# RWKV-style attention and two MLPs on one core: phase 1 without a loop, attention pieces moved

## Chip, cores, metric

One NeuronCore of a Trainium2 chip runs the whole program. The metric is the device time of one execution in microseconds (us), the median over several runs.

## What is computed

Four batches, eight heads, 768 steps, head size 48. The attention is a recurrence over steps, with a decay `w` per channel:

```python
for t in range(S):
    cur = einsum('bhd,bhe->bhde', u * k[t], v[t])
    y[t] = einsum('bhd,bhde->bhe', r[t], state + cur)
    state = w[t][..., None] * state + einsum('bhd,bhe->bhde', k[t], v[t])
x = y as (3072 tokens, 384)
h = x @ w_in                          # 384 x 2048
x = knee(h) @ w_out                   # 2048 x 384; knee: h above 1, 0 below -1, (h+1)^2/4 between
out = (silu(x @ w_gate) * (x @ w_val)) @ w_out2   # 384 x 1536, 1536 x 384
```

## The kernel before

The 3072 tokens are cut into 8 halves (NG = 8; two per batch) of 384 tokens (T), each half into 3 windows of 128. Every large product is taken three times, as hi x hi, hi x lo and lo x hi of operands split into two parts of type fp32r.

**Phase 1** does the first MLP of half g while the attention of half g+1 is woven in. It has 16 slots per half, one for each 128 rows of the hidden layer. In slot j TensorE does `tile_in` of tile j+2 (nine products of 384 columns, line 1042, into PSUM bank `hid[j % 2]`) and `tile_out` of tile j (nine more, line 1066, into `acc`). The tile in between goes through ScalarE (relu and square, lines 701 and 703), VectorE (`gate`, line 926), ScalarE (`ghi`, line 694) and VectorE (`glo`, line 919). In its slot j VectorE does `glo` of tile j+1, `gate` of tile j+2, and then whatever else the slot holds, in that order. `tile_out` waits for `glo` of its tile, and `tile_in` of tile j+4 for `gate` of tile j+2.

**The attention of a half** is a list of 18 pieces, FILLS: for each window KT (k transposed), AT (the products of k and r; two entries, done together), ST (state), Y (output) and XT (output transposed). They use three PSUM banks in turn. WIN_SLOTS puts two entries into each of slots 4 to 12: TensorE does the first between `tile_in` and `tile_out`, the second behind `tile_out`. The next half's `tile_in`, in slot 14, needs all three XT.

Ahead of the pieces stand, on VectorE, the scaling of k and r by the decays (`scale_k`, `scale_r`, lines 856 and 864: 4 instructions in slot 1 and 4 in slot 2) and `diag_sum` (line 868, slot 3). `diag_sum` reads what GpSimd made of r, k and u by two products (`diag_products`, lines 622 and 626); behind it GpSimd does `diag_values` (line 633). The scans of the decays for half g+2 (`scan_pair`, 4 instructions a pair of heads) are VectorE's in slots 9 to 12.

**Loads** are all issued by SyncE, in a fixed order: `load_w(g+2)` when half g+1 is scaled; `load_rest(g+2)` (k and r by channel, then r, k, v by token) when all 18 pieces of half g+1 are done and its y are out; then the store of half g's result. GpSimd's first product waits for r and k by token.

Halves 0 to 5 of phase 1 run in a loop of three rounds of two halves, on every engine (SyncE and GpSimd have loops of their own); halves 6 and 7 are written out. **Phase 2** (the second MLP) has 12 slots per half, with a loop of three rounds of two halves too; it does not change. The attention and the pieces of half 0, with the conversion of the first MLP's weights, come before phase 1.

Of the kernel before, what the change touches and what calls it, by code (L numbers as in the profile page):

```python
# [38 lines left out]
NG = B * S // T  # L39
# [17 lines left out]
NF = len(FILLS)  # L57
# [2 lines left out]
OPS_CHECK = 4  # L60


SCALE_SLOTS = {1: (0, 1), 2: (2, 3)}
DIAG_SLOT = 3
WIN_SLOTS = {4 + i: (2 * i, 2 * i + 1) for i in range(NF // 2)}

CHECK_SLOTS = {5: 0, 6: 1}
SUM_SLOT = 8
SCAN_SLOTS = {9: 0, 10: 1, 11: 2, 12: 3}

CHECK_FILLS = {0: 0, 1: 1}
SCAN_FILLS = {3: 0, 4: 1, 5: 2, 6: 3}
# [10 lines left out]
def build_program(nc, w_d, kd_d, rd_d, rn_d, kn_d, vn_d, u_d, cst_d, w1i_d, w1o_d, w2g_d, w2v_d,  # L83
                  w2o_d, rs_d, ks_d, vs_d, ws_d, us_d, out_d, x2_d, ys_d):
    ctx = ExitStack()
    with ctx:
# [170 lines left out]


        def phase1(e, slot):
            with e.Fori(0, NG // 2 - 1) as b:  # L260
                for hf in range(2):
                    for j in range(J1):
                        slot(b * 2 + hf, j, hf, True, True)
            for g in (NG - 2, NG - 1):
                for j in range(J1):
                    slot(g, j, g % 2, g == NG - 2, False)

        def phase2(e, slot):
            for j in range(J2):
# [208 lines left out]
        def _(e):  # L478
# [65 lines left out]
            def half(g, after_next):  # L544

                if after_next:
                    load_w(g + 2)
                    load_rest(g + 2)
                wait(M["ea", 1], g * 2 + 4)
                wait(M["ed", 1], g + 2)  # L550

                e.dma_start(half_of(x2_d, g), stage[:, :, :]).then_inc(M["st", 1], 16)

            with e.Fori(0, NG // 2 - 1) as b:
                for hf in range(2):
                    half(b * 2 + hf, True)

            wait(fill, NG * NF)
            wait(xl_out, NG * NW)
# [38 lines left out]
        @block.gpsimd  # L598
        def _(e):

            for i in range(2):
                e.memset(att[i][:, :, :], 0.0).then_inc(zero_p, 1)
            e.memset(st[:, :, :], 0.0).then_inc(zero_p, 1)
            e.memset(seed[:, :], 0.0).then_inc(zero_p, 1)

            def split_lo(c, buf, raws, lo, whi_s, wlo_s):
                n = len(raws)
                e.wait_ge(whi_s, c + 1)
                e.wait_ge(raws[c % n], 16 * (c // n + 1))
                e.tensor_tensor(lo[0], buf[:, c % n, :], lo[1].bitcast(F32), ALU.subtract).then_inc(wlo_s, 1)  # L610

            def w1_lo(c):
                if (c + 1) % DVE_LO == 0:
                    return
                t = w1i if c % 2 == 0 else w1o
                split_lo(c, ring, raw, (t[1][:, c // 2, :], t[0][:, c // 2, :]), whi, wlo)

            def diag_products(g):

                e.wait_ge(ld["rn"], (g + 1) * 16)  # L620
                e.wait_ge(ld["kn"], (g + 1) * 16)
                e.tensor_tensor(rk[:, :, :], rk[:, :, :], kn[:, :, :], ALU.mult).then_inc(diag_p, 1)
                e.wait_ge(diag_p, g * 3 + 1)
                e.wait_ge(ld["u"], 16)
                u_b = uu[:, :].rearrange("p (a n) -> p a n", a=1).to_broadcast([P, NW, DM])
                e.tensor_tensor(rk[:, :, :], rk[:, :, :], u_b, ALU.mult).then_inc(diag_p, 1)

            def diag_values(g):

                e.wait_ge(diag_d, g + 1)  # L630
                e.wait_ge(ld["vn"], (g + 1) * 16)
                d_b = dg[:, :, :].rearrange("p w (h o) -> p (w h) o", o=1).to_broadcast([P, NW * H, D])
                e.tensor_tensor(rk[:, :, :].rearrange("p w (h d) -> p (w h) d", d=D),
                                vn[:, :, :].rearrange("p w (h d) -> p (w h) d", d=D), d_b, ALU.mult).then_inc(diag_p, 1)

            for c in range(2 * J1):
                w1_lo(c)
                if c == PRODUCTS_AT:
                    diag_products(0)
                if c == VALUES_AT:  # L640
                    diag_values(0)
            with e.Fori(1, NG) as g:
                diag_products(g)
                diag_values(g)
            for c, (j, s) in enumerate(order2):
                lo = w2o[1][:, j, :] if s == 2 else w2gv(1, j, s)
                hi = w2o[0][:, j, :] if s == 2 else w2gv(0, j, s)
                split_lo(c, ring2, raw2, (lo, hi), whi2, wlo2)
# [3 lines left out]
        def _(e):  # L652
# [91 lines left out]
            def slot(g, j, parity, next_half, after_next):  # L744
                last = isinstance(g, int) and g == NG - 1
                finished, started = nxt(g, j + 1, J1), nxt(g, j + 2, J1)
                if not (last and j + 1 >= J1):
                    hi(1, *finished)
                else:
                    hi(2, 0, 0)  # L750
                if not (last and j + 2 >= J1):
                    knee(*started)
                else:
                    sig(0, j + 2 - J1)
                if next_half:
                    for f in WIN_SLOTS.get(j, ()):
                        drain(g + 1, f, 1 - parity)
                if after_next and j in CHECK_SLOTS:
                    check_w(g + 2, CHECK_SLOTS[j])
                if last and j == 10:  # L760
                    split_x(0, 0)
                if isinstance(g, int) and (last or j > max(WIN_SLOTS)):

                    for _ in range(2 if last and j > 3 else 1):
                        if w2c[0] < W2_EARLY or j >= J1 - 3:
                            w2_hi(w2c[0])
                            w2c[0] += 1
                if j == J1 - 1:
                    copy_out(1, g)
# [53 lines left out]
        def _(e):  # L823
# [64 lines left out]
            def drain(g, f, parity):  # L888
                kind, w, n = FILLS[f]
                src = bank_of(g, f)  # L890
                if kind == "AT":
                    if n == 0:
                        decay_state(g, w, parity)
                    e.wait_ge(ld["cst"], 16)
                    hold(e, "dve", fill, g * NF + (f + 1))
                    mask = later.bitcast(U32).rearrange("p (a t) -> p a t", a=1).to_broadcast([P, 4, WIN])
                    e.copy_predicated(att[n][:, :, :], mask, src[:, :].rearrange("p (a t) -> p a t", a=4))\
                        .then_inc(at_out, 1)
                elif kind == "ST":
                    e.wait_ge(fill, g * NF + (f + 1))  # L900
                    e.wait_ge(st_dec, g * NW + (w + 1))
                    n_pair = state_pairs(w, parity)
                    for i in range(2):
                        r0, c0 = 64 * i, D * i
                        blk = (slice(r0, r0 + D), slice(0, n_pair), slice(c0, c0 + D))
                        ps = src[r0:r0 + D, 0:n_pair * 2 * D].rearrange("p (a c) -> p a c", a=n_pair)[:, :, c0:c0 + D]
                        e.tensor_tensor(st[blk], ps, sbar[blk], ALU.add).then_inc(st_out, 1)
                elif kind == "Y":
                    e.wait_ge(fill, g * NF + (f + 1))
                    e.wait_ge(diag_p, g * 3 + 3)  # L910
                    e.tensor_tensor(xn[:, w, :], src[:, 0:DM], rk[:, w, :], ALU.add).then_inc(y_out, 1)
                elif kind == "XT":
                    e.wait_ge(xh_out, g * NW + (w + 1))
                    e.tensor_tensor(xlo[parity][:, :, cols(w)], src[:, 0:DM].rearrange("p (k t) -> p k t", k=KT),
                                    xhi[parity][:, :, cols(w)].bitcast(F32), ALU.subtract).then_inc(xl_out, 1)
# [117 lines left out]
        def _(e):  # L1033
# [126 lines left out]
            def slot(g, j, parity, next_half, after_next):  # L1160
                last = isinstance(g, int) and g == NG - 1
                if j + 2 < J1:
                    tile_in(g, j + 2, parity)
                elif not last:
                    tile_in(g + 1, j + 2 - J1, 1 - parity)
                else:
                    tile_in2(0, j + 2 - J1, 0)
                fs = WIN_SLOTS[j] if next_half and j in WIN_SLOTS else (None, None)
                if last and j == 4:
                    e.wait_ge(w_sum, NG + 2)  # L1170
                    e.matmul(attb[2][0:1, 0:1], bad[:, OPS_CHECK:OPS_CHECK + 1], ones[:, :], start=True, stop=True).then_inc(w_tot, 1)
                if fs[0] is not None:
                    do_fill(g + 1, fs[0], 1 - parity)
                tile_out(1, g, j, w1o)
                if fs[1] is not None:
                    do_fill(g + 1, fs[1], 1 - parity)

            phase1(e, slot)

# [73 lines left out]
```

## Time and profile before

| | us |
|---|---|
| median of 3 runs | 1057.19 |
| lowest, highest | 1053.92, 1058.22 |
| profiled execution | 1055.94 |
| its span | 1054.1 |
| TensorE busy | 1006.6 (95%) |
| VectorE busy | 547.0 (52%) |
| ScalarE busy | 393.4 (37%) |
| GpSimd busy | 130.2 (12%) |

The span begins with the first instruction and ends with the last; the profiled execution's time has a little around it. PE is TensorE, DVE VectorE, ACT ScalarE, POOL GpSimd, SP SyncE. The granted clock is a share of TensorE's full speed. Phase 1 runs from about 70 to 590 us; half g+1 begins where slot 0's in products follow slot 15's out products. Since the products are pipelined, the distance of their starts tells more than their length.

### The profile page before, as it was taken

The numbers are of one execution on the slowest core, as the hardware profiler recorded it, in microseconds if no ns is written. First come the engines' busy times: TensorE is split into PE (matmuls) and PEld (weight loads), VectorE is DVE, ScalarE is ACT, GpSimd is POOL, SyncE is SP. The second block draws the span as 40 slices with busy tenths as digits, with TensorE's granted clock in tenths as the row PEclk, the third lists the DMA queues.
The fourth block names the chain that finished last, engine by engine and source line by source line (L and its number), as shares of the span: only waits on it lengthen the run. The fifth ranks groups of instructions, "written<-read, shape, count | busy, mean of one in ns | idle before, by whom it ended". The sixth has DMA issues, their size and how long they took to land.

```text
span 1054.1 us, 16811 instructions
## 1 busy us (share of the span) xinstructions
PE 1006.6 (95%) x6162; PEld 992.7 (94%) x6162; DVE 547.0 (52%) x958; ACT 393.4 (37%) x799; POOL 130.2 (12%) x90
## 2 busy tenths in 40 slices
PE   1699999899999999999999999999999999999997
PEld 0689999899999999999999999999999999999997
DVE  7966765556747556577444444333343343434332
ACT  3445354353554444534356532222222222222221
POOL 4650030100200202003015330000000000000000
PEclk9989999899999999999999999999999999999999
DMA  7451130410403104113033220101010101010000
GB/s 226 146 181 27 46 124 2 144 28 1 156 15 120 52 1 142 28 39 105 1 106 100 91 65 14 33 1 46 1 45 0 45 0 45 0 45 0 23 1 25
DMA packets 23200, 59.70 MB, mean 57 GB/s; under 512 B 2656, under 2 KB 11488, under 8 KB 23136
## 3 DMA queue, kind: packets, MB, share of 16 engines
q1 hardware_dynamic: 23136, 58.79, 17.4%
q8 instruction: 47, 0.77, 0.3%
q14 instruction: 17, 0.14, 0.0%
HBM read 49.34 MB, written 9.44 MB: 56 GB/s over the span
## 4 chain that ended last, share of the span: by engine, by line
PE 92%; DVE 2%; issue 2%; DMA 1%; ACT 1%; DVEq 0%; SPq 0%; ACTq 0%
PE bank L1042 48%; PE bank L1066 33%; PE bank L1111 3%; PE bank L1092 2%; PE bank L1107 1%; PE bank L1101 1%; DMA ring<-in_w_out 1%; PE bank L1085 1%; PE bank L1116 1%; DVE suf L834 0%; DVE w_window L839 0%; DVE gate L926 0%; ACT gate L703 0%; ACT gate L701 0%; DVE w1ilo L956 0%
## 5 line engine op out<-in xcount | busy, mean ns | idle before, releaser
L694 ACT ACTIVATE ghi<-gate 128x384 fp32r<-128x384 f32 x224 | 117.3, 523 | 189.2 <-DVE gate L938 95.4
L919 DVE TENSOR_TENSOR glo<-gate,ghi 128x384 fp32r<-128x384 f32 x224 | 136.2, 608 | 87.6 <-ACT ghi L694 85.7
L936 DVE TENSOR_TENSOR gate<-bank,gate 128x384 f32<-128x384 f32 x96 | 53.5, 558 | 220.6 <-ACT gate L798 220.6
L1042 PE MATMUL bank<-xhi,w2gv_alo 128*128 128x384 f32 x480 | 163.2, 340 | 0.0
L1042 PE MATMUL bank<-xhi,w2gv_ahi 128*128 128x384 f32 x480 | 161.8, 337 | 0.0
L1042 PE MATMUL bank<-xlo,w2gv_ahi 128*128 128x384 f32 x480 | 161.8, 337 | 0.0
L1042 PE MATMUL bank<-xhi,w1ihi 128*128 128x384 f32 x384 | 136.4, 355 | 7.7 <-issue 6.5
L1066 PE MATMUL bank<-ghi,w1ohi 128*128 128x384 f32 x384 | 135.7, 353 | 0.5 <-DVE glo L919 0.5
L798 ACT ACTIVATE gate<-bank 128x384 f32<-128x384 f32 x96 | 47.2, 492 | 233.3 <-PE bank L1042 233.3
L1042 PE MATMUL bank<-xhi,w1ilo 128*128 128x384 f32 x384 | 131.6, 343 | 0.0
L1042 PE MATMUL bank<-xlo,w1ihi 128*128 128x384 f32 x384 | 131.6, 343 | 0.0
L1066 PE MATMUL bank<-glo,w1ohi 128*128 128x384 f32 x384 | 130.2, 339 | 0.0
L1066 PE MATMUL bank<-ghi,w1olo 128*128 128x384 f32 x384 | 130.1, 339 | 0.0
L926 DVE SCALAR_TENSOR_TENSOR gate<-bank,gate 128x384 f32<-128x384 f32 x128 | 71.1, 555 | 110.5 <-ACT gate L703 110.3
L701 ACT ACTIVATE gate<-bank 128x384 f32<-128x384 f32 x128 | 62.7, 490 | 151.7 <-PE bank L1042 151.6
L1066 PE MATMUL bank<-ghi,w2olo 128*128 128x384 f32 x288 | 97.9, 340 | 0.0
L1066 PE MATMUL bank<-ghi,w2ohi 128*128 128x384 f32 x288 | 97.1, 337 | 0.0
L1066 PE MATMUL bank<-glo,w2ohi 128*128 128x384 f32 x288 | 97.1, 337 | 0.0
L1042 PEld LDWEIGHTS bank<-xlo,w2gv_ahi 128*128 128x128 f32 x480 | 90.2, 188 | 0.0
L1042 PEld LDWEIGHTS bank<-xhi,w2gv_ahi 128*128 128x128 f32 x480 | 90.1, 188 | 0.0
L1042 PEld LDWEIGHTS bank<-xhi,w2gv_alo 128*128 128x128 f32 x480 | 90.1, 188 | 0.0
L1042 PEld LDWEIGHTS bank<-xhi,w1ihi 128*128 128x128 f32 x384 | 73.7, 192 | 9.6 <-issue 7.1
(81 smaller groups left out, 1598.6 us busy)
## 6 DMA issues: line engine op xcount, KB each, us to landing
w_by_channel<-in_w_channel SPq DMA_DIRECT2D x16, 339.5 KB, 3.9
k_by_channel<-in_k_channel SPq DMA_DIRECT2D x16, 336.0 KB, 4.7
r_by_channel<-in_r_channel SPq DMA_DIRECT2D x16, 336.0 KB, 5.5
ring<-in_w_out SPq DMA_DIRECT2D x28, 192.0 KB, 2.8
r_k_diag<-in_r_token SPq DMA_DIRECT2D x8, 576.0 KB, 6.7
k_by_token<-in_k_token SPq DMA_DIRECT2D x8, 576.0 KB, 8.4
v_by_token<-in_v_token SPq DMA_DIRECT2D x8, 576.0 KB, 9.4
x_t<-ring SPq DMA_DIRECT2D x8, 576.0 KB, 3.5
```

Source lines behind the costliest of these rows:

```text
L694: e.activation(ghi[j % 2][:, :], gate[j % 2][:, :], ACT.Copy).then_inc(M["hi", ph], 1)
L701: e.activation(q, hid[j % 2][:, 0:T], ACT.Relu, bias=0.5, scale=0.5).then_inc(M["q", 1], 1)
L798: e.activation(gate[j % 2][:, :], hid[j % 2][:, 0:T], ACT.Sigmoid).then_inc(M["q", 2], 1)
L919: e.tensor_tensor(glo[j % 2][:, :], gate[j % 2][:, :], ghi[j % 2][:, :].bitcast(F32), ALU.subtract)\
L926: e.scalar_tensor_tensor(q, hid[j % 2][:, 0:T], 1.0, q, ALU.max, ALU.min).then_inc(M["g", 1], 1)
L936: e.tensor_tensor(q, hid[j % 2][:, 0:T], q, ALU.mult).then_inc(M["t", 2], 1)
L1042: m = e.matmul(out, w_of(a, k), x_of(b_, k), start=start and i == 0, stop=stop and i == total - 1)
L1066: m = e.matmul(acc[k][:, 0:T], wo[a][:, j, k * P:(k + 1) * P], gs[b_][:, :], start=(j == 0 and i == 0), stop=(j == J[ph] - 1 and i == 2))
L1085: m = e.transpose(out[:, p * PR:(p + 1) * PR], kd[:, p, cols(w)], ident[0:PR, 0:PR])
L1092: m = e.matmul(o[:, p * WIN:(p + 1) * WIN], kd[r, p, cols(w)], rd[r, p, cols(w)], start=True, stop=True)
L1101: m = e.matmul(out[0:PR, p * 2 * D:(p + 1) * 2 * D], ktk[w % 2][:, p * PR:(p + 1) * PR], vn[:, w, p * 2 * D:(p + 1) * 2 * D], start=True, ...
L1111: m = e.matmul(out[:, h * D:(h + 1) * D], att[h % 2][:, h // 2, :], vn[:, w, h * D:(h + 1) * D], start=(row_start and h == 0), stop=(h == ...
```

## The change

The loop of phase 1 is written out on all engines, so waits become constants. The two entries of a slot now both stand between `tile_in` and `tile_out`. The pieces move up by one slot, to slots 3 to 11, but for the last entry, XT of window 2, which stays in slot 12 (now ahead of `tile_out`). The scaling moves to slots 0 and 1, `diag_sum` to slot 2, the scans to slots 10, 12, 13 and 14.

```diff
--- before.py
+++ after.py
@@ -60,13 +60,14 @@
 OPS_CHECK = 4
 
 
-SCALE_SLOTS = {1: (0, 1), 2: (2, 3)}
-DIAG_SLOT = 3
-WIN_SLOTS = {4 + i: (2 * i, 2 * i + 1) for i in range(NF // 2)}
+SCALE_SLOTS = {0: (0, 1), 1: (2, 3)}
+DIAG_SLOT = 2
+WIN_SLOTS = {3 + i: (2 * i, 2 * i + 1) for i in range(NF // 2)}
+WIN_SLOTS[11], WIN_SLOTS[12] = (NF - 2,), (NF - 1,)
 
 CHECK_SLOTS = {5: 0, 6: 1}
 SUM_SLOT = 8
-SCAN_SLOTS = {9: 0, 10: 1, 11: 2, 12: 3}
+SCAN_SLOTS = {10: 0, 12: 1, 13: 2, 14: 3}
 
 CHECK_FILLS = {0: 0, 1: 1}
 SCAN_FILLS = {3: 0, 4: 1, 5: 2, 6: 3}
@@ -257,13 +258,9 @@
 
 
         def phase1(e, slot):
-            with e.Fori(0, NG // 2 - 1) as b:
-                for hf in range(2):
-                    for j in range(J1):
-                        slot(b * 2 + hf, j, hf, True, True)
-            for g in (NG - 2, NG - 1):
+            for g in range(NG):
                 for j in range(J1):
-                    slot(g, j, g % 2, g == NG - 2, False)
+                    slot(g, j, g % 2, g < NG - 1, g < NG - 2)
 
         def phase2(e, slot):
             for j in range(J2):
@@ -551,9 +548,8 @@
 
                 e.dma_start(half_of(x2_d, g), stage[:, :, :]).then_inc(M["st", 1], 16)
 
-            with e.Fori(0, NG // 2 - 1) as b:
-                for hf in range(2):
-                    half(b * 2 + hf, True)
+            for g in range(NG - 2):
+                half(g, True)
 
             wait(fill, NG * NF)
             wait(xl_out, NG * NW)
@@ -639,7 +635,7 @@
                     diag_products(0)
                 if c == VALUES_AT:
                     diag_values(0)
-            with e.Fori(1, NG) as g:
+            for g in range(1, NG):
                 diag_products(g)
                 diag_values(g)
             for c, (j, s) in enumerate(order2):
@@ -759,7 +755,7 @@
                     check_w(g + 2, CHECK_SLOTS[j])
                 if last and j == 10:
                     split_x(0, 0)
-                if isinstance(g, int) and (last or j > max(WIN_SLOTS)):
+                if last or (g == NG - 2 and j > max(WIN_SLOTS)):
 
                     for _ in range(2 if last and j > 3 else 1):
                         if w2c[0] < W2_EARLY or j >= J1 - 3:
@@ -891,8 +887,9 @@
                 if kind == "AT":
                     if n == 0:
                         decay_state(g, w, parity)
-                    e.wait_ge(ld["cst"], 16)
-                    hold(e, "dve", fill, g * NF + (f + 1))
+                    if g == 0:
+                        e.wait_ge(ld["cst"], 16)
+                    e.wait_ge(fill, g * NF + (f + 1))
                     mask = later.bitcast(U32).rearrange("p (a t) -> p a t", a=1).to_broadcast([P, 4, WIN])
                     e.copy_predicated(att[n][:, :, :], mask, src[:, :].rearrange("p (a t) -> p a t", a=4))\
                         .then_inc(at_out, 1)
@@ -1165,15 +1162,13 @@
                     tile_in(g + 1, j + 2 - J1, 1 - parity)
                 else:
                     tile_in2(0, j + 2 - J1, 0)
-                fs = WIN_SLOTS[j] if next_half and j in WIN_SLOTS else (None, None)
                 if last and j == 4:
                     e.wait_ge(w_sum, NG + 2)
                     e.matmul(attb[2][0:1, 0:1], bad[:, OPS_CHECK:OPS_CHECK + 1], ones[:, :], start=True, stop=True).then_inc(w_tot, 1)
-                if fs[0] is not None:
-                    do_fill(g + 1, fs[0], 1 - parity)
+                if next_half:
+                    for f in WIN_SLOTS.get(j, ()):
+                        do_fill(g + 1, f, 1 - parity)
                 tile_out(1, g, j, w1o)
-                if fs[1] is not None:
-                    do_fill(g + 1, fs[1], 1 - parity)
 
             phase1(e, slot)
```

## Rows read from the trace of the kernel before

**Rows 1.** The page's first part: busy time, share of the span, instructions.
```profile
PE 1006.6 (95%) x6162; PEld 992.7 (94%) x6162; DVE 547.0 (52%) x958; ACT 393.4 (37%) x799; POOL 130.2 (12%) x90
```

**Rows 2.** Waits of TensorE: who waited for whom, total us, times, longest.
```profile
PE bank L1042 <- issue: 6.5, 2, 3.3
...
PE bank L1066 <- DVE glo L919: 0.5, 1, 0.5
```

**Rows 3.** The chain that ended last: start us, us, what, how many.
```profile
589.85 3.16 PE bank L1042 x18
```

**Rows 4.** Timeline of TensorE at the loop's two jumps: start, us, instruction.
```profile
200.26 0.34 PE L1066 MATMUL bank<-ghi,w1ohi 128*128 128x384 f32 x1
...
211.09 0.34 PE L1042 MATMUL bank<-xhi,w1ihi 128*128 128x384 f32 x1
...
339.14 0.34 PE L1066 MATMUL bank<-ghi,w1ohi 128*128 128x384 f32 x1
...
348.86 0.34 PE L1042 MATMUL bank<-xhi,w1ihi 128*128 128x384 f32 x1
```

**Rows 5.** Stretches: window, busy by engine, granted clock, DMA share, GB/s.
```profile
198.00:202.00 4.00, 4.00 (x23) 3.68 (x21) 1.58 (x3) 1.96 (x4) 0.00 (x0) 1.00 1.03 369
205.00:208.00 3.00, 2.72 (x8) 2.73 (x9) 0.00 (x0) 0.00 (x0) 2.92 (x2) 0.50 0.21 79
470.00:480.00 10.00, 10.00 (x59) 10.00 (x58) 6.12 (x12) 5.49 (x12) 0.00 (x0) 1.00 0.98 290
```

**Rows 6.** Timeline of TensorE behind an attention piece (KT0, half 2).
```profile
150.19 0.42 PE L1066 MATMUL bank<-ghi,w1ohi 128*128 128x384 f32 x1
150.45 0.33 PE L1066 MATMUL bank<-glo,w1ohi 128*128 128x384 f32 x1
```

**Rows 7.** Timeline of TensorE and GpSimd, half 0 to 1.
```profile
125.80 0.49 PE L1116 MATMUL bank<-cst,x_by_token 128*128 128x128 f32 x3
126.04 0.42 PE L1042 MATMUL bank<-xhi,w1ihi 128*128 128x384 f32 x1
...
137.70 2.68 POOL L622 TENSOR_TENSOR r_k_diag<-r_k_diag,k_by_token 128x1152 f32<-128x1152 f32 x1 [50.71 <-DMA k_by_token<-in_k_token]
```

**Rows 8.** Timeline of all engines in the first slots of phase 1.
```profile
71.77 0.56 DVE L926 SCALAR_TENSOR_TENSOR gate<-bank,gate 128x384 f32<-128x384 f32 x1 [0.38 <-ACT gate L703]
72.06 2.69 POOL L622 TENSOR_TENSOR r_k_diag<-r_k_diag,k_by_token 128x1152 f32<-128x1152 f32 x1 [9.70 <-DMA k_by_token<-in_k_token]
...
73.00 2.17 DVE L919 TENSOR_TENSOR glo<-gate,ghi 128x384 fp32r<-128x384 f32 x1 [0.67 <-ACT ghi L694]
...
74.83 2.88 POOL L626 TENSOR_TENSOR r_k_diag<-r_k_diag,u_rows 128x1152 f32<-128x1152 f32 x1
...
76.23 0.34 PE L1066 MATMUL bank<-ghi,w1ohi 128*128 128x384 f32 x1
...
80.06 0.45 PE L1066 MATMUL bank<-ghi,w1ohi 128*128 128x384 f32 x1 [0.50 <-DVE glo L919]
```

**Rows 9.** Timeline of all engines, half 5 to 6, in written-out code.
```profile
468.93 0.42 PE L1042 MATMUL bank<-xhi,w1ihi 128*128 128x384 f32 x1
...
481.46 2.69 POOL L622 TENSOR_TENSOR r_k_diag<-r_k_diag,k_by_token 128x1152 f32<-128x1152 f32 x1 [52.19 <-DMA k_by_token<-in_k_token]
...
484.23 2.88 POOL L626 TENSOR_TENSOR r_k_diag<-r_k_diag,u_rows 128x1152 f32<-128x1152 f32 x1
...
485.02 2.51 DVE L856 TENSOR_TENSOR k_by_channel<-k_by_channel,suf 112x384 f32<-112x384 f32 x1
...
488.87 0.54 DVE L919 TENSOR_TENSOR glo<-gate,ghi 128x384 fp32r<-128x384 f32 x1
...
489.60 0.34 PE L1066 MATMUL bank<-ghi,w1ohi 128*128 128x384 f32 x1
```

**Rows 10.** Timeline of VectorE around one scan.
```profile
121.41 0.96 DVE L834 TENSOR_TENSOR_SCAN suf<-w_by_channel,cst 112x387 f32<-112x387 f32 x1
...
123.71 0.53 DVE L919 TENSOR_TENSOR glo<-gate,ghi 128x384 fp32r<-128x384 f32 x1
```


## The prediction, as it went on record

> **What bounds the kernel now.** I read the page's busy line first: TensorE is busy 95% of the span, VectorE 52% [rows 1]. So only what TensorE waits for, or how fast it is clocked, can move the time. The list of its waits then shows, apart from the start-up, two waits put down to "issue", 6.5 us together, 3.3 the longer, and one of 0.5 us for `glo` [rows 2]. The timeline of TensorE shows the rest: 18 products of 384 columns take 3.16 us, 0.1757 us each [rows 3], and a slot of phase 1 (nine in, nine out) is 3.17 us wherever no attention piece stands. Outside those three waits the stream is closed. So the change can gain in two places only, at the two jumps of phase 1's loop and at the seams between kinds of products; it can lose wherever VectorE, moved earlier, hands over late.
>
> **The loop's two jumps.** Slot 15's out products of an odd half start at 200.26; the in products of slot 1 start at 211.09 [rows 4]. That is 10.83 us for nine out products (1.58) and one slot (3.17), 4.75 us of work: 6.08 us lost. At the second jump, 339.14 to 348.86: 9.72 - 4.75 = 4.97 us lost. Part is the idle itself, part the half-speed stream behind it: the granted clock was 0.50 from 205 to 208 [rows 5], that is the 1.2 GHz level, where it had been 2.4 GHz before the idle. Written out, halves 0 to 5 are the same kind of code as halves 6 and 7 are now, which show no such gap. Term: -11.05 us.
>
> The Trainium skill, "Runtime: NRT & Kernel Launch", section "Instruction fetch mechanics", says that a taken branch to code that isn't loaded stalls until the code is fetched, and advises unrolling. By that rule all loop jumps stall; the trace agrees at phase 1's two, but phase 2's loop, which stays a loop, shows no such wait [rows 2]. By the rule the sum would be this term's -11.05, and nothing more to be had here.
>
> **Both pieces at one place.** The first large product behind small ones starts 0.26 us before the next (150.19 to 150.45) where 0.1757 is usual [rows 6]: 0.08 us for each return. Pieces that now stand together (KT0 with AT0, KT1 with Y0, XT0 with ST1, KT2 with Y1, XT1 with ST2) save one return each: 5 in each of 7 halves, 35 x 0.08 = -2.8 us. The bounds: 0, if small products of unlike shape cost each other the same, and -6, if the 0.09 us ahead of a piece goes as well. I take -2.8, since only the return is a row. The waits inside the pairs are covered: the closest, ST1 and ST2, need the bank of the AT piece of the slot before, which ends 3.5 us ahead of them (an out and an in group and XT lie between); VectorE copies it out straight after that slot's `gate` instruction, in half that time.
>
> **Scaling in slots 0 and 1: the cost.** SyncE may load k and r of the next-but-one half once the last transposes are done, and these move from behind slot 12's out products to ahead of them. The transposes start 0.24 us before slot 13 now (125.80 against 126.04) [rows 7]; then they have an out group of 1.66 us behind them: loads and all that hangs on them come 1.67 us earlier. But the scaling, 4 VectorE instructions a slot, comes a whole slot, 3.17 us, earlier. Between the two stand GpSimd's two products of r, k and u, 2.7 and 2.9 us long, the first from 137.70 [rows 7], the second straight behind it, to 143.35. While one runs, a VectorE instruction with two SBUF tensors does not: `glo` took 2.17 us in place of 0.56 at 73.00, beside the product of 72.06 [rows 8], and a scaling took 2.51 beside the one of 484.23, ending 0.42 us after it [rows 9].
>
> Now: the second product of the last transition ends at 484.23 + 2.88 = 487.11; the first scaling ends at 487.53, three more (0.47 each) and `glo` follow, `glo` ends at 489.42, and the out products that need it start at 489.60 [rows 9]: 0.2 us to spare; by the same count 1.0 in the first transition. New: the product ends 1.67 us earlier, at 485.44; the same four scalings and `glo` then end 2.30 us later, at 487.74, but what they hold up is the out group of slot 2, due a slot earlier, at 486.43. TensorE waits 487.79 - 486.43 = 1.36 us. For the first transition the same count (products start 11.66 us after slot 13 instead of 12.53) gives 0.49. There are six such transitions; with starts 11.66, 11.64, 12.16, 11.56, 11.64 and 12.53 us behind slot 13 (the first and the last of them are shown, [rows 7, 9]) the sum is 0.49 + 0.47 + 0.99 + 0.39 + 0.47 + 1.36 = +4.2 us. At two of them the loop's stall hides this now. Bounds: 0, if landings come 1 us earlier, and +10, if 1 us later.
>
> **Start-up.** Half 1's loads are issued by the same event as before, so the products run at 72.06 and 74.83 again [rows 8]. Slot 0's second `gate` instruction ends at 72.33, and now a scaling follows at 72.24. It is caught by the first product and ends at 75.16 (as `glo` did); the second product gets in (74.83, 2.88 us), the next scaling is caught too and ends at 78.12; two more, then `glo` for slot 2, to 79.52. Its out group starts at 79.56, not 76.23: 3.33 us. The wait that stands at 80.06 now (0.66 us with its tail) goes, since pieces stand ahead of that out group. Net +2.7 us.
> TensorE then has been idle 3.15 us. Both idles of 3.2 to 3.3 us at the jumps were followed by a slow stream: of the 11.05 us, 6.5 are idle and 0.3 the last product's usual tail, so half clock cost 4.2 us in two [rows 2, 4, 5]. I take it that it does here too, +2.1; bounds 0 and 2.7.
>
> The Trainium skill, "SBUF — State Buffer", section "SBUF: two separate sides", calls the port pair that VectorE and GpSimd share an exclusive lock, held for the whole instruction. The rows above agree (2.17 us for 0.56). Without the lock, start-up and transitions would cost nothing and the sum would be -13.85; the page does not say who gets the next turn, on which a rival rests.
>
> **What else moves.** Y2 and XT2 now stand a slot apart instead of around one out group; no wait stood there, so nothing is gained beyond the earlier load. Scans go to slots 10, 12, 13, 14. A pair's scan takes VectorE 2.3 us (121.41 to 123.71) [rows 10], with `glo` and `gate` (0.47 each) 3.24 us in a slot of 3.17: it falls behind 0.2 us over three slots where I count 1.4 us to spare for `glo`. Nothing. Queued behind VectorE's wait for `diag_p` in slot 2 would be `glo` of slot 4, but the products end 3 us before. SyncE's w load goes out a slot earlier, onto idle queues; its loop, like VectorE's, ScalarE's and GpSimd's, was not what TensorE waited for.
>
> **Sum.** -11.05 - 2.8 + 4.2 + 2.7 + 2.1 = -4.9 us. Against the profiled execution (1055.94 us, of which the span is 1054.1): 1051.1. The median of the three runs is 1.25 us above it, so 1052.3.
>
> **Rivals.**
> (a) The clock does not fall at start-up: the idle is slightly shorter than the two that were followed by it. -7.0 us, 1050.2.
> (b) VectorE keeps its turn while its scalings stand back to back, and the second product waits. Then `glo` of slot 2 ends at 77.04, TensorE waits 0.9 us instead of 3.3, the clock stays: start-up +0.2. -9.5 us, 1047.7. For it: no row has two such VectorE instructions in a row beside a waiting product. Against: the product of 74.83 queued behind the end of one `glo` (75.17) and had it all to itself at once, ending at 77.71 [rows 8].
> (c) Landings 1 us later: in the written-out code other transfers sit differently. Six waits grow by 1 us each: +1.1 us, 1058.3. For it: the spread of the landings is 1 us. Against: five of six agree within 0.6.
> (d) Slower: the gap at the two jumps is not the jump, but code that comes late while the load burst fills the DMA engines, which the written-out code would meet as well. The burst ran just before both (share 1.03 at 198 to 202) [rows 5]. Then -11.05 goes, the two waits there (0.86) stay hidden: -2.8 + 3.3 + 2.7 + 2.1 = +5.3 us, 1062.5. It decides if even one 5 us gap is left at each of those two places. Against: the same burst at 470 to 480 (0.98), in written-out code, with no gap [rows 5].
>
> **Chances.** Forecast 0.42, (a) 0.18, (b) 0.20, (c) 0.12, (d) 0.08. A measurement of this kernel tells about 0.5% (5.3 us) from no change. The forecast, 4.9 us down, stands just inside: I give 0.17 of its 0.42 to faster. Of (a) 0.15, of (b) all 0.20: faster 0.52. Slower has 0.05 from (d) and 0.01 from (c): 0.06. Same: 0.42. Range 1046.5 to 1057.5: down to (b) with a larger saving at the seams, up to most of (c).
>
> **What would show it.** No "issue" wait near 200 and 340, and granted clock 1.00 there. Five new TensorE waits for `glo`, or six, of 0.4 to 1.4 us, at the out group of slot 2 of each half from the second. One of 3.2 us near 76, with half clock behind it. Two VectorE scalings of over 2.5 us there (one only: (b)). The first out product behind a pair of pieces still 0.26 us, but five fewer of them in a half. Wrong would be: waits in slots 3 to 12, GpSimd's products starting at another distance than 10.0 to 10.9 us from slot 13, or a gap for "issue" in written-out code.

## The result and the profile after

The changed kernel takes 1050.87 us (median of 11 runs, 1048.61 to 1052.95), the one before 1056.6 (1053.1 to 1058.9): ratio 0.9951, 95% interval 0.9938 to 0.9965, 5.2 us less by the ratio. The profiled execution has a span of 1048.6 us.

The waits of TensorE after (who waited for whom: total us, times, longest), to set against [rows 2]:

```profile
PE bank L1082 <- DVE r_by_channel L860: 23.1, 4, 10.3
PE bank L1113 <- DVE x_by_token L908: 7.8, 2, 6.2
PE bank L1063 <- DVE glo L916: 3.1, 2, 2.9
```

The two waits for "issue" are gone, and the wait for `glo` has grown from 0.5 to 3.1 us. (The first two lines are the start-up, there before as well.) Where the first jump was, now the change of halves at 205.0, the stream is closed and fast; stretches, with granted clock, DMA share and GB/s at the end, against [rows 5]:

```profile
198.00:202.00 4.00, 4.00 (x24) 4.00 (x23) 3.83 (x9) 1.87 (x4) 0.00 (x0) 1.00 1.01 294
202.00:205.00 3.00, 3.00 (x19) 3.00 (x19) 2.90 (x6) 1.55 (x3) 0.23 (x1) 1.00 0.88 353
205.00:208.00 3.00, 3.00 (x19) 3.00 (x19) 2.53 (x5) 2.31 (x5) 2.92 (x2) 1.00 0.40 158
```

The long wait for `glo` stands where [rows 8] stood. The timeline of GpSimd, VectorE and TensorE after:

```profile
72.15 2.69 POOL L618 TENSOR_TENSOR r_k_diag<-r_k_diag,k_by_token 128x1152 f32<-128x1152 f32 x1 [9.65 <-DMA k_by_token<-in_k_token]
72.55 2.71 DVE L852 TENSOR_TENSOR k_by_channel<-k_by_channel,suf 112x384 f32<-112x384 f32 x1
...
74.92 2.85 POOL L622 TENSOR_TENSOR r_k_diag<-r_k_diag,u_rows 128x1152 f32<-128x1152 f32 x1
75.18 3.00 DVE L860 TENSOR_TENSOR r_by_channel<-r_by_channel,w_by_channel 112x384 f32<-112x384 f32 x1
...
79.04 0.55 DVE L916 TENSOR_TENSOR glo<-gate,ghi 128x384 fp32r<-128x384 f32 x1
...
79.64 0.44 PE L1063 MATMUL bank<-ghi,w1ohi 128*128 128x384 f32 x1 [2.90 <-DVE glo L916]
```

Two scalings of 0.55 us took 2.71 and 3.00, each caught behind one product; `glo` of slot 2 came at 79.59 and the out products started at 79.64, due at 76.57. The clock did not fall behind this wait: it is 1.00 from 80 to 83.

At the first half change (where half 0 gives way to half 1), against [rows 7, 9]:

```profile
138.60 2.69 POOL L618 TENSOR_TENSOR r_k_diag<-r_k_diag,k_by_token 128x1152 f32<-128x1152 f32 x1 [52.03 <-DMA k_by_token<-in_k_token]
...
139.83 1.87 DVE L916 TENSOR_TENSOR glo<-gate,ghi 128x384 fp32r<-128x384 f32 x1 [0.46 <-ACT ghi L690]
141.37 2.88 POOL L622 TENSOR_TENSOR r_k_diag<-r_k_diag,u_rows 128x1152 f32<-128x1152 f32 x1
...
142.09 2.57 DVE L852 TENSOR_TENSOR k_by_channel<-k_by_channel,suf 112x384 f32<-112x384 f32 x1
...
144.63 0.34 PE L1039 MATMUL bank<-xhi,w1ihi 128*128 128x384 f32 x1
...
146.59 0.44 PE L1063 MATMUL bank<-ghi,w1ohi 128*128 128x384 f32 x1 [0.22 <-DVE glo L916]
```

The out group was due 1.58 us behind 144.63, at 146.21, and started at 146.59. At the five later changes the same place loses 0.04 to 0.08 us and about 0.1 in the longer first product.

Taken apart by the starts of slot 0's in products (first seven halves, us each, from the timelines of TensorE; "in all" begins at phase 1's very first product, 5.3 us ahead of slot 0 before and 5.1 us after; the last column is the pitch, the distance from one slot's start to the next):

| | half 0 | 1 | 2 | 3 | 4 | 5 | 6 | phase 1 in all | phase 2, us a slot |
|---|---|---|---|---|---|---|---|---|---|
| before | 67.31 | 69.66 | 69.22 | 69.57 | 68.22 | 66.22 | 66.58 | 526.70 | 4.740 |
| changed | 69.65 | 66.68 | 66.71 | 66.43 | 66.71 | 66.39 | 66.69 | 519.03 | 4.752 |

Phase 1 is 7.7 us shorter. Of that 1.6 us is lost again from phase 2's start on, 1.2 of it because every one of the 96 slots is 0.012 us longer with the same instructions (see "Open" below), and 0.6 ahead of phase 1. That leaves 5.5 us, the difference of the two spans.

### The profile page after: what moved, and what is told of

The parts are those of the page before. It is cut to its first block, busy times and chain, and to the rows that moved or that the text cites. A ratio compares the mean times of both kernels' runs of the same rounds, so it can differ in the third digit from the quotient of the medians.

```text
span 1048.6 us, 15818 instructions
## 1 busy us (share of the span) xinstructions
PE 1004.0 (96%) x6162; PEld 990.1 (94%) x6162; DVE 555.8 (53%) x958; ACT 394.5 (38%) x799; POOL 133.6 (13%) x90
## 4 chain that ended last, share of the span: by engine, by line
PE 92%; DVE 4%; issue 1%; ACT 1%; DMA 1%; SPq 0%; DVEq 0%; ACTq 0%
PE bank L1039 47%; PE bank L1063 34%; PE bank L1108 4%; PE bank L1089 2%; PE bank L1104 2%; PE bank L1098 1%; PE bank L1082 1%; PE bank L1113 1%; DVE w_window L835 1%; DVE r_by_channel L860 1%; DVE k_by_channel L852 1%; DVE suf L830 1%; DVE w_by_channel L843 0%; DMA w_by_channel<-in_w_channel 0%; DMA ring<-in_w_out 0%
## 5 line engine op out<-in xcount | busy, mean ns | idle before, releaser
L1039 PE MATMUL bank<-xhi,w1ihi 128*128 128x384 f32 x384 | 130.7, 340 | 1.3 <-DVE xlo L911 1.3
L1063 PEld LDWEIGHTS bank<-ghi,w1ohi 128*128 128x128 f32 x384 | 72.2, 188 | 7.4 <-DVE glo L916 4.8
```

Of the source, the lines that this page charges most:

```text
L1039: m = e.matmul(out, w_of(a, k), x_of(b_, k), start=start and i == 0, stop=stop and i == total - 1)
L1063: m = e.matmul(acc[k][:, 0:T], wo[a][:, j, k * P:(k + 1) * P], gs[b_][:, :], start=(j == 0 and i == 0), stop=(j == J[ph] - 1 and i == 2))
```

## Experiments

Each ran beside the kernel before on the same chip; ratios are to that.

**1. Only written out** (`e1_written_out`): the kernel before, with this and the same for SyncE and GpSimd (and VectorE's wait for an AT piece as a constant).

```diff
-            with e.Fori(0, NG // 2 - 1) as b:
...
-            for g in (NG - 2, NG - 1):
+            for g in range(NG):
                 for j in range(J1):
-                    slot(g, j, g % 2, g == NG - 2, False)
+                    slot(g, j, g % 2, g < NG - 1, g < NG - 2)
```

> The kernel before with phase 1 written out on all engines and nothing moved. Theory A (the jumps alone give the gain; the moves cost): the two gaps for issue and the half clock behind them go, 11.05 us; no new wait for glo, only the 0.5 us one near 80 stays: 11 us under before, 1045.6 if before is 1056.6, and 4 to 5 us under the changed kernel. Theory B (written-out code alone is worth what the changed kernel shows, the moves are neutral): 5.7 us under before, 1051. Theory C (the moves bring the gain): no change, or gaps for issue remain.

Measured: 1045.37 us, ratio 0.9905 (0.9889 to 0.9921), phase 1 in all 515.27 us, halves 67.55, then 66.22 and 66.54 in turn (one of the latter is 66.61). Its wait of TensorE in phase 1:

```profile
PE bank L1062 <- DVE glo L915: 0.6, 1, 0.6
```

Theory A holds. The four halves around the two jumps (1 to 4) are 11.1 us shorter than in the kernel before; by the medians the gain is 10.0 us. Phase 1 in all is 11.4 us shorter, but 0.5 of that lies ahead of slot 0, in the first products, which take 4.8 to 5.8 us from run to run. Everything else in the change costs 3.4 us of the seven halves.

**2. Only moved** (`e2_moved_only`): the changed kernel with the loops put back.

> The changed kernel with its loops put back: only the moves. Theory A: both gaps for issue stand as before; the wait near 76 is 2.9 us (2.4 more than before); at the four half changes without a jump 0.2 to 1 us each; the seams give nothing: 3.5 to 6 us over before. Theory of the prediction's seam term (2.8 us saved by both pieces at one place): 1 to 3 us over. Theory C (the moves gain): below before.

Measured: 1059.64 us, ratio 1.0043 (1.0027 to 1.006): slower than before. Its waits:

```profile
PE bank L1043 <- issue: 5.3, 2, 2.9
PE bank L1067 <- DVE glo L920: 3.9, 3, 3.3
```

The moves alone make the kernel slower by 4 to 5 us, as theory A had it. (Its nine runs lie between 1056.83 and 1062.41 us; the profile is of one in the lower half, with a span only 1.8 us over that of before. In it the two jumps idle 2.9 and 2.4 us, and only the first is followed by half clock.)

**3. Both pieces at one place** (`e3_one_place`): `e1_written_out` and this.

```diff
-                if fs[0] is not None:
-                    do_fill(g + 1, fs[0], 1 - parity)
+                for f in WIN_SLOTS.get(j, ()):
+                    if f < NF - 1:
+                        do_fill(g + 1, f, 1 - parity)
                 tile_out(1, g, j, w1o)
+                if next_half and j == max(WIN_SLOTS):
+                    do_fill(g + 1, NF - 1, 1 - parity)
```

> As e1_written_out, and both pieces of a slot ahead of the out products, but no slot changed (Y and XT of window 2 still around the out products of slot 12). Prediction's term: 35 seams of 0.08 us go, 2.8 us under e1_written_out. Theory A (two unlike small pieces cost each other the same 0.08 us): within 0.5 us of e1_written_out, and the first piece of a pair 0.08 us longer in the timeline.

Measured: 1044.81 us, ratio 0.9901 (0.9884 to 0.9919), no different from experiment 1; halves 1 to 6 are 66.23 and 66.55 us in turn, against 66.22 and 66.54. The seams gave nothing. (Half 0 is 0.8 us shorter, since the wait of 0.6 us for `glo` is gone; phase 1 in all, 515.53 against 515.27, hides that behind slower first products.) The timeline of TensorE around KT0 and AT0 in this kernel shows why:

```profile
149.62 0.55 PE L1081 MATMUL bank<-cst,k_by_channel 112*128 112x112 f32 x4
150.09 1.16 PE L1088 MATMUL bank<-r_by_channel,k_by_channel 48*128 48x128 f32 x16
```

KT to AT is 0.47 us, where the out product followed 0.31 us behind KT before. So the seam between two small pieces costs 0.16 us, as much as the return (0.08 us) and the approach (0.09 us) that the pair saves together. The expectation's theory A had 0.08 for it.

**4. GpSimd's products behind the scaling** (`e4_products_later`): the changed kernel and this.

```diff
-DIAG_SLOT = 2
+DIAG_SLOT = 4
...
             def diag_products(g):
+                if g > 0:
+                    e.wait_ge(scaled, (g + 1) * (2 * NPAIR))
                 e.wait_ge(ld["rn"], (g + 1) * 16)
```

> The changed kernel, with GpSimd's two products for the next half made to wait until VectorE has scaled that half, and the sum over them in slot 4 instead of 2. Theory A (the new waits are VectorE's scalings caught behind GpSimd's products): the wait of 2.9 us near 76 and the six small ones at the half changes vanish, 3.5 us under the changed kernel, about 1047.3. Rival (VectorE simply has too much to do in slots 0 and 1, whoever runs beside it: eight scalings of 0.47 us): the wait near 76 stays over 1.5 us and the time is that of the changed kernel, 1050.9.

Measured: 1046.0 us, ratio 0.9913 (0.9898 to 0.9927); phase 1 515.26 us, halves 66.52, 66.26, 66.58, 66.26, 66.58, 66.26, 66.58; no wait for `glo` at all. With the same eight scalings in slots 0 and 1, it is the products beside them that cost: 3.1 us in half 0, 1.1 in the next six together (the halves of the changed kernel less these). Without that cost the rearranged kernel is as fast as experiment 1's, and no faster: the moves by themselves gain nothing.

**5. More products** (`e11_twice_the_products`): the changed kernel and, behind the two products,

```diff
+                if g > 0:
+                    for i in range(2):
+                        e.wait_ge(more_p, (g - 1) * 2 + i)
+                        e.tensor_tensor(kn[:, :, :], kn[:, :, :], u_b, ALU.mult).then_inc(more_p, 1)
```

> The changed kernel with two more GpSimd products of the same size behind the two of each half but the first (into a tile that nobody reads any more). Theory A with turns taken one by one: each of the next two scalings is caught as well, 3.0 us in place of 0.47: the wait near 76 grows from 2.9 to about 8 us, and each of the six half changes waits about 5 us, 35 to 40 us over the changed kernel (more where the clock falls). If VectorE kept its turn once it has it: no scaling but the first is caught, and nothing is added.

Measured: 1096.08 us in one run, 45 over. Its waits, the scalings at the first half change (the four products start at 143.02, 145.79, 148.64 and straight behind it), and the stretch behind:

```profile
PE bank L1068 <- DVE glo L921: 31.9, 7, 5.0
PE bank L1087 <- DVE r_by_channel L865: 24.3, 5, 9.8
```

```profile
146.51 2.58 DVE L857 TENSOR_TENSOR k_by_channel<-k_by_channel,suf 112x384 f32<-112x384 f32 x1
149.02 3.01 DVE L865 TENSOR_TENSOR r_by_channel<-r_by_channel,w_by_channel 112x384 f32<-112x384 f32 x1
151.95 2.96 DVE L857 TENSOR_TENSOR k_by_channel<-k_by_channel,suf 112x384 f32<-112x384 f32 x1
```

```profile
156.00:159.00 3.00, 3.00 (x10) 3.00 (x11) 3.00 (x7) 1.43 (x3) 0.00 (x0) 0.52 0.00 0
```

Each half change waits 4.75 to 4.96 us, and each is followed by half clock, 1.4 to 2.6 us more, which makes up what the expectation lacked. One scaling gets in between two products; rival (b) falls here as in the rows of the changed kernel. The 8 us expected near 76 did not come: the extra products caught scalings of slot 1 instead (two waits, 3.2 and 1.9 us).

**6. Which jumps cost.** Phase 1's loop jumps stalled, phase 2's did not. Five kernels on it. First, phase 2's loop written out too (`e7_phase2_written_out`, the same edit in `phase2`):

> e1_written_out with phase 2 written out too. By the rule that every loop jump stalls: some us under e1_written_out. By the trace of before, which shows no wait at phase 2's two jumps: within 1 us of it, 0.990 of before.

Measured: 1045.85 us, ratio 0.9901 (0.9882 to 0.9921); halves and pitch as in experiment 1. Phase 2's jumps cost nothing.

Theory S of the next expectations is that the length of the loop's body decides, theory Q that the lead does: how far TensorE's sequencer, which hands the instructions on, is ahead of the products when it comes to the jump. A longer body for phase 2's loop (`e6_longer_body`, `e1_written_out` and this):

```diff
             def slot2(g, j, parity, last=False):
+                if not isinstance(g, int):
+                    for _ in range(48):
+                        e.wait_ge(M["h", 1], 1)
```

(two waits make one instruction.)

> e1_written_out, with 24 more instructions a slot in the body of phase 2's loop on TensorE's sequencer (waits on a count long reached): its body grows from some 1350 instructions to some 1920, as long as phase 1's was. Theory S (a jump costs when the loop's body is long; phase 1's loop was, phase 2's isn't): two gaps of 3 us for issue appear in phase 2, near 745 and 860, with half clock behind them, 8 to 11 us in all over e1_written_out. Theory Q (a jump costs where the sequencer has no lead: phase 2's slots give more lead, whatever the body's length): no gap over 1 us.

Measured: 1057.83 us in one run. Its waits, and the timeline of TensorE at the first jump of phase 2:

```profile
PE bank L1038 <- issue: 7.0, 2, 3.6
```

```profile
759.67 0.33 PE L1062 MATMUL bank<-ghi,w2olo 128*128 128x384 f32 x1
763.64 0.57 PE L1038 MATMUL bank<-xhi,w2gv_ahi 128*128 128x384 f32 x1 [3.63 <-issue]
764.01 0.52 PE L1038 MATMUL bank<-xlo,w2gv_ahi 128*128 128x384 f32 x1
```

From the start of the last out group to the next in group it is 5.37 and 5.17 us in place of 1.58, and the in groups behind take 4.80 in place of 3.16: 3.8 + 3.6 us at the gaps and 2 x 1.6 of half clock, 10.6 us. These are the gaps of phase 1's jumps, made in phase 2 by the padding alone.

A shorter body for phase 1's loop (`e8_shorter_body`, the kernel before and this; one of three products of each out group is left out in the loop):

```diff
-                    for i, (a, b_) in enumerate(THREE):
+                    three = THREE[:2] if ph == 1 and not isinstance(g, int) else THREE
+                    for i, (a, b_) in enumerate(three):
...
```

> The kernel before, with one product in three of the out groups left out in phase 1's loop (part of the sum of the first MLP's output is missing in halves 0 to 5): the body shrinks from some 1900 to some 1700 instructions, and a slot from 3.17 to 2.64 us, so the sequencer's lead shrinks too. Theory S: both gaps for issue vanish or shrink to below 1 us. Theory Q: both stay at 3 us or grow. Either way phase 1 is 50 us shorter (96 slots x 0.53).

Measured: 1030.06 us in one run, some 26 us less in place of 50, since with shorter slots TensorE waits 9.1 us for `glo`, and longer at pieces and jumps. The gaps stay and grow:

```profile
PE bank L1042 <- issue: 8.9, 2, 4.5
```

By itself this spoke for theory Q. Two more kernels decided. Little lead at the jump (`e9_no_lead`, `e1_written_out` and this in phase 2):

```diff
+                if not isinstance(g, int) and parity == 0 and j == J2 - 1:
+                    e.wait_ge(M["h", 2], (g + 1) * J2 + 2)
                 tile_out(2, g, j, w2o)
```

> e1_written_out, with one wait more in phase 2's loop: ahead of its last out group TensorE's sequencer waits until the in products before it are done, so that it reaches the jump 1.6 us before the work it has handed on runs out, where it could be 4 us ahead or more. The body stays at some 1350 instructions. Theory Q (a jump costs where the sequencer has no lead): two gaps of 2 to 4 us for issue near 760 and 875. Theory S (it costs only where the body is long): 0.2 us each, for the wait itself.

Measured: 1047.85 us in one run, no wait for issue; in each of the three rounds the last in group is 0.21 us longer, the wait itself, and the out group behind it 0.1. And a body in between (`e10_half_as_long`, 20 waits in place of 48):

> As e6_longer_body with 10 instructions a slot in place of 24: a body of some 1590. e6 showed gaps of 3.6 and 3.4 us at 1920, e8 of 4.5 us at some 1700 (in phase 1). Theory S with a limit between 1590 and 1700: no gap. With a limit between 1350 and 1590: gaps of over 3 us again. Theory Q: a gap that shrinks with the padding, about 1 us or none.

Measured: 1047.11 us in one run, no gap. (Theory Q allowed that too; it is the run before that refutes it.) So:

| kernel, loop | instructions in the body | lead | idle at a jump, us |
|---|---|---|---|
| before, phase 2 | ~1350 | as it is | 0 |
| e9, phase 2 | ~1350 | at most 1.6 us | 0 |
| e10, phase 2 | ~1590 | with 10 more instructions a slot | 0 |
| e8, phase 1 | ~1700 | shorter slots | 4.5, 4.4 |
| before, phase 1 | ~1900 | as it is | 3.3, 3.2 |
| e6, phase 2 | ~1920 | with 24 more instructions a slot | 3.6, 3.4 |

(Bodies are counted from the products in the trace, each with its weight load: 892 in a round of phase 1 before, 796 in e8, 648 in phase 2, with some 110 others in phase 1's loop and 50 in phase 2's, and the padding, 240 in e10 and 576 in e6.) In phase 2's loop a smaller lead does not make the jump stall, and a longer body does, from somewhere between some 1590 and some 1920 instructions of TensorE. If phase 1's loop has the same limit, e8 puts it below some 1700. Whether the lead sets how long a stall lasts, as e8's longer gaps suggest, is not shown. The Trainium skill, "Runtime: NRT & Kernel Launch", section "Instruction fetch mechanics", gives TensorE an instruction memory of 2048 instructions, refilled in blocks of 256. The runs have a stall at some 1900 already, and with e8 (an estimate) the limit lies 1.4 to 1.8 such blocks below 2048.

**7. The changed kernel again** (`after_again`).

> The changed kernel once more. If the pitch of phase 2's slots (4.752 us in its trace, 4.740 in those of before, e1, e2 and e3, with the same instructions) belongs to the execution, it can come out as 4.740 here, and the span is 1.1 us shorter; if it belongs to the kernel, it is 4.752 again. Time 0.995 of before either way.

Measured: 1052.17 us, ratio 0.9965 (0.995 to 0.998): 3.7 us less than the kernel before, where the first series had 5.2. The span of the profiled execution is 1053.4. The pitch is 4.75 again. Of the 4.8 us that the span is longer than in the first profile 4.1 are in phase 1, 2.5 of them in its first half and 1.0 at the half changes:

```profile
PE bank L1063 <- DVE glo L916: 3.3, 2, 2.5
```

```profile
80.00:83.00 3.00, 2.51 (x8) 2.51 (x9) 3.00 (x7) 1.43 (x3) 0.00 (x0) 0.50 0.00 0
```

The wait near 76 is 2.5 us, shorter than before, and yet the clock fell behind it: the next out and in groups took 3.05 and 2.88 us, 2.7 more than in the first profile. The last half change waits 0.8 us, at the out group of slot 0: there a scan of slot 14 was caught behind GpSimd's first product, and `glo` came late.

```profile
473.77 3.31 DVE L843 TENSOR_TENSOR_SCAN w_by_channel<-w_by_channel,scan_seed 112x387 f32<-112x387 f32 x1
```

## Why the prediction was right, and where it was not

Forecast 1052.3, measured 1050.87; 4.9 us down forecast, 5.2 by the ratio (3.7 in experiment 7). That the sum comes out so near is in good part luck: the seams are 2.8 us too good in it, the half changes 2.1 to 3.1 and in the first profile the clock 2.1 too bad, and some 2 us were lost outside the seven halves, which no term had.

| step | predicted | measured | by |
|---|---|---|---|
| two jumps | -11.05 | -11.1 | experiment 1, halves 1 to 4 |
| seams | -2.8 | 0 | experiment 3 |
| six half changes | +4.2 | +1.1 and +2.1 | changed kernel, twice, against experiment 4 |
| start-up | +2.7 | +2.3 | 69.65 against 67.31 |
| clock behind it | +2.1 | 0 and +2.7 | profile after, experiment 7 |
| ahead of phase 1, and from phase 2 on | none | +0.6 and +1.6 | profile after |

**Jumps**: right in place and price; only the reason was left at "a jump". It is the jump of a loop whose body is too long. From the Trainium skill's section on instruction fetch the prediction took that all loop jumps stall; phase 2's, free in the kernel before, e9 and e10, show that they do not.

**Seams**: the step failed. The return behind a piece costs 0.08 us, as read, but I took it that two small pieces side by side don't cost each other anything. They cost 0.16 us (experiment 3), as much as is saved; the bound of 0 was the value. No row stood for it, and I chose the end that the nearest rows seemed to favour.

**Half changes**: the mechanism was right, the size not, and one of the prediction's own signs of being wrong came: the products started 8.5 to 9.8 us behind slot 13, not 10.0 to 10.9; of the six waits for `glo` at slot 2 only the first is listed, with 0.22 us. Two rows of SyncE's timeline after show a part of it: the seven loads were issued within 2.7 us (3.4 at one change), where the loop needed 3.0 to 4.0 (126.53 in the kernel before to 130.55, the longest):

```profile
127.44 0.31 SPq L494 DMA_DIRECT2D k_by_channel<-in_k_channel  x1
...
130.15 0.43 SPq L489 DMA_DIRECT2D v_by_token<-in_v_token  x1
```

I moved the queue's start and not its pace. Experiment 1, written out and nothing moved, has the same pace, and its products start 10.4 to 12.0 us behind slot 13, where before they start at 11.6 to 12.5; experiment 2, moved and in the loop, has 9.2 to 10.2. (The loop's waits are for values in registers, those of the written-out code for constants; that this makes the pace is not shown by itself.) Being earlier, the first product met VectorE's scan of slot 14, and waited for it and for the `glo` behind it:

```profile
336.83 0.96 DVE L843 TENSOR_TENSOR_SCAN w_by_channel<-w_by_channel,scan_seed 112x387 f32<-112x387 f32 x1
337.14 3.65 POOL L618 TENSOR_TENSOR r_k_diag<-r_k_diag,k_by_token 128x1152 f32<-128x1152 f32 x1 [50.53 <-DMA k_by_token<-in_k_token]
337.71 0.54 DVE L916 TENSOR_TENSOR glo<-gate,ghi 128x384 fp32r<-128x384 f32 x1
```

3.65 us in place of some 2.65: it ends at 340.79, 2.6 us after `glo` gives way to the next VectorE instruction at 338.16. So the second product ended 15.1 us behind slot 13 in five of six changes, whatever the landing, just early enough. For the scans the prediction has "Nothing.", and this is the other side of it: they cost TensorE nothing in the first profile, and held GpSimd. (In experiment 7 one of them did cost, 0.8 us.)

**Start-up**: right to 0.4 us, with its two caught scalings. **Clock**: forecast and rival (a) each came true once; it differs between executions, and what decides it is not shown.

**Rivals**: (b) is refuted by the rows at 72.55 and 75.18 and by experiment 5; (c) went the other way; (d) fell with experiment 1. What the prediction did not say is that the kernel it forecast was worse than one half of the change: written out alone it is 4.9 us faster, by the ratios (0.9905 against 0.9951).

**Open**: the pitch of phase 2's slots is 4.740 us in the kernel before, e1, e2, e3, e7, e8 and e10, and 4.75 in the changed kernel (twice), e4, e6, e9 and e11, with every product 0.4 ns longer and no wait. That is 1.2 us of the changed kernel's time. It is not the chip (e1 to e4 ran on one), and it followed the kernel the one time that could be tested (experiment 7), but I have no cause for it.

## What to carry to other kernels

Write out a loop, or cut its body, when the trace shows a gap for issue at its jump, and look at each loop by itself: of two loops in this kernel one cost 5.5 us a jump and the other nothing. When work is moved to an earlier slot, ask what runs beside it there: here the same eight instructions cost nothing or 4 to 8 us (with the clock), depending on whether two GpSimd instructions stood behind or among them. And price the parts of a change apart: this one gained 10 to 11 us with one part and gave 5 to 6 back with the others.

## What the runs showed of the hardware

- A loop jump on TensorE is free with a body of some 1350 and some 1590 instructions (before, e9, e10) and costs 2.4 to 4.5 us idle with some 1700 and more (before, experiment 2, e6, e8), at seven of the eight jumps with 1.4 to 2.9 us of half clock behind it.
- VectorE instructions with two SBUF tensors, the scans among them, and GpSimd's products exclude each other for the whole instruction. Between scalings they took turns one by one: 0.55 us became 2.7 to 3.0 twice in a row. But a product that came during a scan let the `glo` behind it go first as well, and took 3.65 us in place of some 2.65 (337.14; 3.47 at 470.41).
- The granted clock does not follow the length of the idle alone. Waits of 2.5 us (experiment 7) and 4.75 to 4.96 us (experiment 5, six of six) were followed by the 1.2 GHz level, waits of 2.9 (changed kernel) and 3.3 us (experiment 2) were not. In e8 a wait of 1.92 us (at 79.55) was, one of 1.93 (at 142.97) was not.
- Going from one small piece to another of unlike shape costs 0.16 us at the seam (KT to AT, experiment 3), as much as from large products to small ones and back together (0.09 and 0.08 us).
